# Forming one step's low-half weights on POOL instead of DVE in a two-layer mixture-of-experts kernel

## What is computed

```python
def _attn_ref(x, f_logit, lower_bound):
    ...
    for t in range(S):
        h = f[:, t] * h + i[:, t] * x[:, t]
        y[:, t] = h
...
    for e in range(E):          # both mixture-of-experts layers, 8 experts
        mask = expert_idx == e
        ...
        h = np.maximum(x[mask] @ w1[e], 0.0)
        out[mask] = gate_w[mask, None] * (h @ w2[e])
```

## Time and profile before

| | us |
|---|---|
| median of 3 runs | 1242.16 (1241.43 to 1242.8) |
| the profiled execution's own time | 1241.81 |
| its span | 1240.1 |
| PE busy in the span | 1199.8 (97%) |
| DVE busy | 967.9 (78%) |
| ACT busy | 816.7 (66%) |
| POOL busy | 423.3 (34%) |

### The profile page before, as it was taken

How to read it: one execution, slowest core, us unless ns; L and a number is a source line. 1 busy time by engine, 2 the same in 40 slices (tenths; PEclk the granted TensorE clock), 3 DMA queues, 4 the chain that set the end, 5 groups by cost and what they waited for, 6 DMA issues and landing times.

```text
span 1240.1 us, 28252 instructions
## 1 busy us (share of the span) xinstructions
PE 1199.8 (97%) x9957; PEld 1163.7 (94%) x9957; DVE 967.9 (78%) x1585; ACT 816.7 (66%) x1436; POOL 423.3 (34%) x436
## 2 busy tenths in 40 slices
PE   6999699999999999999999999999999999999997
PEld 6997459999999999999999999999999999999996
DVE  5877938888877777789877788988777777788885
ACT  4775357778766666666666666566666666577774
POOL 3665022232321121223222143434454443435331
PEclk9998899999999999999999999999999999999998
DMA  7999839888866766779777668666766666678880
GB/s 263 331 314 337 169 27 306 259 281 275 268 221 216 240 220 218 224 220 180 244 231 228 218 214 211 218 206 206 221 218 222 227 220 207 220 257 274 264 273 18
DMA packets 202373, 284.21 MB, mean 229 GB/s; under 512 B 39478, under 2 KB 165060, under 8 KB 202276
## 3 DMA queue, kind: packets, MB, share of 16 engines
q1 hardware_dynamic: 189892, 249.84, 66.1%
q0 software_dynamic: 12384, 33.10, 7.6%
HBM read 250.48 MB, written 33.33 MB: 229 GB/s over the span
## 4 chain that ended last, share of the span: by engine, by line
PE 84%; DVE 9%; issue 3%; ACT 2%; POOL 1%; ACTq 0%; DVEq 0%; POOLq 0%
PE bank L1720 36%; PE bank L1699 32%; PE bank L1691 3%; PE bank L1668 3%; PE bank L1579 2%; PE bank L1544 2%; PE bank L1525 2%; PE bank L1538 1%; PE bank L1693 1%; PE bank L1565 1%; DVE hT L514 1%; DVE w1l L481 1%; ACT w1h L1294 1%; PE bank L1603 1%; DVE gx L504 1%
## 5 line engine op out<-in xcount | busy, mean ns | idle before, releaser
L1699 PE MATMUL bank<-xs,w1h 128*128 128x256 f32 x2496 | 461.0, 283 | 2.4 <-DVE h_sum L885 1.6
L1720 PE MATMUL bank<-w2h,hh 128*128 128x264 f32 (+1 forms) x1376 | 392.4, 285 | 0.4 <-DVE hl L892 0.4
L1720 PE MATMUL bank<-w2l,hh 128*128 128x264 f32 (+1 forms) x1376 | 389.5, 283 | 0.0
L1720 PE MATMUL bank<-w2h,hl 128*128 128x264 f32 (+1 forms) x1376 | 388.3, 282 | 0.0
L1699 PEld LDWEIGHTS bank<-xs,w1h 128*128 128x128 f32 x2496 | 380.8, 188 | 3.3 <-DVE xs L873 1.3
L1441 ACT ACTIVATE hh<-bank 128x512 fp32r<-128x512 f32 x312 | 186.3, 597 | 274.3 <-PE bank L1699 273.7
L1699 PE MATMUL bank<-xs,w1l 128*128 128x256 f32 x1248 | 348.5, 279 | 0.0
L892 DVE SCALAR_TENSOR_TENSOR hl<-bank,hh 128x512 fp32r<-128x512 f32 x312 | 215.2, 690 | 111.0 <-ACT hh L1441 108.2
L481 DVE TENSOR_TENSOR w1l<-w1raw,w1h 128x1024 fp32r<-128x1024 f32 x188 | 230.3, 1225 | 49.9 <-ACT w1h L1294 48.8
L489 DVE TENSOR_TENSOR w2l<-w2raw,w2h 128x1024 fp32r<-128x1024 f32 x188 | 230.6, 1226 | 37.3 <-ACT w2h L1302 34.9
L1720 PEld LDWEIGHTS bank<-w2h,hh 128*128 128x128 f32 x1376 | 259.0, 188 | 0.6 <-DVE hl L892 0.6
(11 more groups left out here) (213 smaller groups left out, 1210.8 us busy)
## 6 DMA issues: line engine op xcount, KB each, us to landing
w1raw<-in_moe_w SPq DMA_DIRECT2D x94, 1024.0 KB
w2raw<-in_moe_w SPq DMA_DIRECT2D x94, 1024.0 KB, 5.8
rows_b<-yb SPq DMA_DIRECT2D x86, 128.0 KB, 2.5
xin<-in_x SPq DMA_DIRECT2D x19, 512.0 KB, 5.5
fin<-in_f_logit SPq DMA_DIRECT2D x19, 512.0 KB, 6.6
rows_a<-h_rows SPq DMA_DIRECT2D x19, 512.0 KB, 5.3
w_stage<-in_moe_w SPq DMA_DIRECT2D x12, 512.0 KB, 8.0
wgraw<-gates_d SPq DMA_DIRECT2D x46, 32.0 KB, 5.3
```

The source lines that it names most:

```text
L1699: ins = mm(bank[j % UB][:, f * GW:(f + 1) * GW], w[p][:, o:o + P], xs[:, p, a, c * GW:(c + 1) * GW], start=k == 0, stop=k == 3 * DC - 1)
L1720: ins = mm(bank[Y_BANK + rows_slot(i, t)][:, 0:n], a[:, j, o:o + P], w[p][:, 2 * j + f, 0:n], start=(j, f, k) == (0, 0, 0), stop=(j, f, k) ...
```

## The change

The low halves of `w1` for step 1 (two pieces of 128x1024) are formed by POOL. DVE skips them in step 0. POOL has them behind its first two gathers and `places` of step 2, ahead of the step loop, each behind a wait for ACT's high half. As both engines now add to `w1_lo`, DVE waits for the count of 4 ahead of its pieces for step 2. All other weights are formed as before.

```diff
@@ split_w1_lo (DVE) @@
                 wait(dve, w1_hi, i.value(2, c + 1))
+                if i.var is None and i.const == 2:
+                    dve.wait_ge(w1_lo, 4)
@@ step (DVE) @@
-                    hidden_beside(i, 0, lambda: split_w1_lo(nxt, 0))
+                    hidden_beside(i, 0, lambda: split_w1_lo(nxt, 0) if i.var is not None or i.const > 0 else None)
...
-                    hidden_beside(i, 1, lambda: split_w1_lo(nxt, 1))
+                    hidden_beside(i, 1, lambda: split_w1_lo(nxt, 1) if i.var is not None or i.const > 0 else None)
@@ gpsimd @@
             places(Index(2))
+
+            for c in range(DC):
+                cols = slice(c * F, (c + 1) * F)
+                pool.wait_ge(w1_hi, 2 + c + 1)
+                pool.tensor_tensor(w1l[1][:, cols], w1raw[:, 1, cols], w1h[1][:, cols].bitcast(fp32),
+                                   ALU.subtract).then_inc(w1_lo, 1)
             tick = beside(resort(0), resort(1))
```

## The result

The changed kernel is slower by a little: median 1243.97 us (1241.68 to 1247.11, 20 runs) against 1241.28 us for the kernel before (1239.65 to 1242.8, 20 runs). The ratio is 1.0024 with a 95% interval of 1.0016 to 1.0031, or +3.0 us (2.0 to 3.8); the two medians themselves differ by 2.7 us. The forecast was 1242.9 us, +0.8 us, and no change beyond 0.2%. The time lies in the range, but the shift is more than three times the forecast, and at 0.24% it lies at the edge of the 0.2%, more likely beyond it than within.

A forecast was written before the change was run, and what follows sets the result against it. The prediction took PE, released by step 0's DVE and ACT chain, as the bound: -1.53 us removed and +2.3 us for a late gather gave +0.8 us, 1242.9 us, range 1240.6 to 1245.0.

The forecast's parts named there:

- The chain in step 0: Start of step 1: work on DVE and ACT from 182 us, through DVE's weight split, releases PE at 195.47 us.
- handover: PE's matmul group at 195.47 us, after which PE runs without a gap; forecast to move by +0.8 us, and the end equally.
- What the two splits cost on DVE's chain: Step 0 on DVE: without two subtractions of 1.22 us, quarter 2's xs and h_sum come 1.53 us earlier, handover at 193.94.
- What is added to POOL: Step 0: two subtractions, stretched by three quarters of DVE neighbours' time, end at 188.4 us; covered up to 189.1.
- POOL's own price: POOL in step 0: 1.7 ns a column, so 1.95 us for each 1024-column piece without a DVE neighbour.
- The gather is late: Step 2's gather, issued at 188.6 us, lands 7.3 us later at 195.9; PE waits some 3 us, handover +2.3 us.
- The sign: Slower by 0.8 us: the late gather's +2.3 us outweighs the 1.53 us removed; wrong if the landing takes under 5 us.
- Rival 1: Step 2's gather takes turns with weight loads, lands at 192 before PE comes; full 1.53 us gain, 1240.6 us; chance 0.22.
- Rival 2: POOL in step 0 takes 2.6 to 2.9 us a piece; handover +1.6 to +2.4 us, 1243.7 to 1244.6; chance 0.18.
- Rival 3: TensorE's clock falls between 193 and 199 us in PE's hole, costing 1.7 us more, 1244.6 us or above; chance 0.14.

## Why the prediction was right or wrong

- **The chain in step 0 bounds the start of step 1, and its handover to PE sets the end: right.** The span ends 1044.5 to 1044.6 us behind the handover in the kernel before and in five others, and 1.5 us more in the two where the clock fell behind it. In three it is 0.4 to 0.9 us more without a fall behind the handover; there PE waits 0.5 to 1.0 us longer for DVE's `vals` much later, which no edit here aimed at. The run with the loads held back is not counted.
- **What the two splits cost on DVE's chain, 1.53 us: right in size, but POOL does not give it back.** The other order on DVE gave 1.5 us. In the changed kernel h_sum of quarter 2 came 1.7 us late instead.
- **What is added to POOL: the step that failed.** I read two rows in which POOL was slow beside DVE, and concluded that DVE's operations with two SBUF inputs slow POOL by three quarters of their time; a loss of DVE's did not stand in the sum. I never asked for the other direction: a short DVE operation that comes while POOL is at work. It waits until POOL's 2.34 us are over. The prediction even cited the Trainium skill's statement that such DVE instructions contend with GpSimd (GPSIMD Engine Reference, 1 Specifications), and charged all of it to POOL. Another page of the Trainium skill states the rule that I needed (SBUF — State Buffer, SBUF: two separate sides): of a DVE instruction with two SBUF inputs and a GpSimd instruction that reads SBUF, whichever starts first has the shared port pair for its whole instruction, and the other is fully blocked. The rows at 183.80 and 183.89, the held hl and meta, the h_sum that is not held, and the POOL piece of 1.75 us behind a DVE split all agree; only that a POOL operation that is held lost 0.75 to 0.8 of DVE's time in the three cases here, and not all of it. One row does not as it stands: at 12.28 us POOL's record starts 0.04 us ahead of DVE's, and POOL is the one that is stretched. Which of two starts so close together counts as the first, no run here tells.
- **POOL's own price, 1.95 us a piece: too low, and made good by luck.** It is 2.36 us, 2.3 ns a column. The rows I extended from have a broadcast operand and 1.7 ns. The Trainium skill's figure (GPSIMD Engine Reference, 3.1 Elementwise), as an estimate 2.25 us a piece, was nearer. But the 0.4 and 0.3 us that I added for DVE's neighbours did not come, so the two pieces took 4.7 us in all where the sum had 4.6.
- **The gather is late and PE waits for it: right, with its landing.** 7.67 us against 7.3 taken. Its issue was off, 190.56 instead of 188.6, and nearly all of these 2.0 us is the hold on DVE: POOL's second piece could begin only at 188.04 instead of 186.2. With the 0.4 us of the landing this takes the handover from +0.8 to +2.9. PE's hole was 2.05 us and not 3, because PE was late too: its step 1 began at 190.90, released by h_sum, and not at 188.45, released by POOL.
- **The sign and the number.** The sign came out for the reason given, as the gather ends last. The hold on DVE would have turned it without any gather, by 1.7 us, and that was not in the prediction. The number, 1242.9 against 1243.97 us, looks better than the shift because the three runs that it started from had a median 0.9 us above that of all 20 (1242.16 against 1241.28). That is luck. Slower by more than 0.2%, where the ratio of 1.0024 points, had a chance of 0.15.
- **Rival 1, that the gather shares the engines and lands in time: excluded.** Issued behind the weight loads it landed after 6.8 to 8.1 us in five profiles. It would have followed from the Trainium skill's statement that each engine takes its queues in turns (DMA: Bandwidth & Descriptors, Queues, rings and completion order); the landings of this case do not bear that out.
- **Rival 2, POOL slower than my rows: its numbers come near, its mechanism did not happen.** It had a landing at 196.7 to 197.5 and +1.6 to +2.4 us, measured are 198.2 and +2.9. But its pieces of 2.6 to 2.9 us took 2.34 and 2.37; the delay was a hold on DVE and not a slow POOL.
- **Rival 3, the fall of the clock: it happened,** near the place named, in the profiled execution and, by the spread of the times, in about eight of 20 runs. Its 1.7 us were 1.5. With a chance of 0.14 it was put too low. Why it falls in one execution and not in another stays open.

## What to carry to other kernels

Before work goes from DVE to POOL, look at what DVE does at the same time. In these traces the DVE operations that read two SBUF tensors, and the fp32 copy within SBUF, waited until POOL's running subtraction was over, so a short one on the critical chain paid for a long one off it. Ask next what stands behind the new work in POOL's queue; a gather that moved from an idle DMA stretch to one with 2 MB of loads under way landed 5 us later here. And where a split stands ahead of a sum that others wait for, first try the other order on the same engine: here it gave the whole gain of 1.5 us for nothing.

## What the runs showed of the hardware

- Beside a POOL subtraction over 1024 columns a DVE subtraction of 64 columns took 2.33 us (0.22 alone), hl of 256 columns 2.60 (0.42), and a copy of 4 columns 1.35 (0.16). With an input in PSUM DVE was not held (0.43 us beside POOL). Cut in pieces of 256 columns, POOL held the 64 columns for one piece only (0.72 us in all).
- The other way round, a POOL piece of 256 columns took 1.75 us (0.74 alone) while a DVE split of 1.23 us ran.
- An indirect gather of one tile landed after 2.7 us with the DMA engines idle, after at most 3.8 with the weight loads held back (one execution), and after 6.8 to 8.1 behind them (five profiles).
- In the changed kernel the granted clock fell to its lower level (0.50) at 199.2 us, behind 6.3 us in which PE was busy for 3.7, with a last hole of 2.05 us, and came back at 202.6. In other profiles it fell behind a hole of 1.47 us and stayed up behind one of 2.50.
